# Moving the token-side sums of the down product and the last loads and stores before it in a fused attention and MoE kernel

## The reference

```
def _moe2_ref(x, w_in, w_out) -> np.ndarray:
    h = x @ w_in
    g = np.maximum(0.01 * h, h)
    return (g @ w_out).astype(np.float32)
```

## Time and profile before

| what | value |
|---|---|
| median of 3 runs | 822.38 us (821.12 to 822.7) |
| the profiled execution's own time | 823.07 us |
| its span in the trace | 821.2 us |
| PE busy | 805.5 us, 98% |
| DVE busy | 546.6 us, 67% |
| ACT busy | 457.7 us, 56% |
| POOL busy | 98.1 us, 12% |
| granted clock of PE over the span | 0.997 |
| DMA | 156.64 MB, mean 191 GB/s |

### The profile page before, as it was taken

How to read it: one execution, slowest core, us unless ns; L and a number is a source line. 1 busy time by engine, 2 the same in 40 slices (tenths; PEclk the granted TensorE clock), 3 DMA queues, 4 the chain that set the end, 5 groups by cost and what they waited for, 6 DMA issues and landing times.

```text
span 821.2 us, 13098 instructions
## 1 busy us (share of the span) xinstructions
PE 805.5 (98%) x4844; PEld 659.0 (80%) x4844; DVE 546.6 (67%) x906; ACT 457.7 (56%) x737; POOL 98.1 (12%) x220
## 2 busy tenths in 40 slices
PE   8889999999999999999999999999989999999998
PEld 6677778787888888888888888888868888888886
DVE  7778988877743285527643335665788699769775
ACT  4567777767743346345565446566744554555553
POOL 4454445432210000000000000000000000000000
PEclk9999999999999999999999999999999999999999
DMA  9675768665758876246684568445931840373002
GB/s 345 229 274 171 219 197 234 183 191 123 213 198 235 306 264 244 102 174 206 232 289 168 183 221 295 154 155 170 375 145 55 294 166 26 100 266 122 27 1 77
DMA packets 84496, 156.64 MB, mean 191 GB/s; under 512 B 6737, under 2 KB 35537, under 8 KB 84433
## 3 DMA queue, kind: packets, MB, share of 16 engines
q1 hardware_dynamic: 84432, 155.81, 56.6%
HBM read 99.16 MB, written 56.62 MB: 190 GB/s over the span
## 4 chain that ended last, share of the span: by engine, by line
PE 90%; DMA 3%; DVE 2%; issue 1%; POOL 1%; SPq 0%; ACT 0%; POOLq 0%; DVEq 0%
PE hid_a L731 22%; PE hid_b L731 21%; PE attn_ps L731 13%; PE scores_a L731 13%; PE scores_b L731 8%; PE probs_ps L731 7%; PE attn_ps L723 3%; DMA q_raw<-q_in 2%; DMA g_blk<-g_scratch 2%; PE probs_ps L709 2%; PE scores_a L697 1%; PE scores_b L697 1%; DVE ring_lo L1145 1%; DVE g_blk L1293 1%; POOL attn_buf L1435 0%
## 5 line engine op out<-in xcount | busy, mean ns | idle before, releaser
L862 ACT ACTIVATE ring_hi<-g_blk 128x512 fp32r<-128x512 f32 x168 | 105.9, 632 | 111.8 <-PE hid_a L731 42.5
L1145 DVE TENSOR_TENSOR ring_lo<-g_blk,ring_hi 128x512 fp32r<-128x512 f32 x168 | 115.2, 688 | 35.9 <-ACT ring_hi L862 32.6
L1009 ACT ACTIVATE g_out<-g_out 128x512 f32<-128x512 f32 x72 | 45.4, 630 | 71.4 <-DVE g_out L1272 41.1
L731 PE MATMUL hid_b<-ring_hi,w_hi 128*128 128x512 f32 x128 | 49.9, 390 | 0.2 <-DVE ring_lo L1145 0.2
L731 PE MATMUL hid_b<-ring_hi,w_lo 128*128 128x512 f32 x128 | 49.8, 389 | 0.0
L731 PE MATMUL hid_b<-ring_lo,w_hi 128*128 128x512 f32 x128 | 49.8, 389 | 0.0
L731 PE MATMUL hid_a<-w_in_hi,xT_hi 128*128 128x512 f32 x96 | 39.9, 416 | 4.0 <-DVE u L1191 3.3
L1145 DVE TENSOR_TENSOR w_lo<-w_raw,w_hi 128x1792 fp32r<-128x1792 f32 (+2 forms) x24 | 33.6, 1401 | 8.7 <-ACT w_hi L862 8.6
L731 PE MATMUL hid_b<-w_in_hi,xT_hi 128*128 128x512 f32 x96 | 39.3, 409 | 0.0
L1145 DVE TENSOR_TENSOR x_op_P_lo<-op_raw,x_op_P_hi 128x1024 fp32r<-128x1024 f32 x21 | 25.7, 1224 | 19.8 <-ACT x_op_P_hi L862 19.7
L901 ACT ACTIVATE u<-u,shift,gain 128x1024 f32<-128x1024 f32 x24 | 29.8, 1240 | 15.9 <-POOL shift L1455 15.8
(11 more groups left out here) (205 smaller groups left out, 2158.6 us busy)
## 6 DMA issues: line engine op xcount, KB each, us to landing
g_scratch<-g_out SPq DMA_DIRECT2D x96, 256.0 KB, 2.6
g_blk<-g_scratch SPq DMA_DIRECT2D x48, 512.0 KB, 7.2
attn_buf<-k_in SPq DMA_DIRECT2D x32, 384.0 KB, 5.6
attn_buf<-v_in SPq DMA_DIRECT2D x32, 384.0 KB, 3.9
ln_scratch<-lnT SPq DMA_DIRECT2D x24, 512.0 KB, 6.0
w_raw<-w_in SPq DMA_DIRECT2D x16, 512.0 KB, 4.2
q_raw<-q_in SPq DMA_DIRECT2D x32, 192.0 KB, 5.0
ln_even<-ln_scratch SPq DMA_DIRECT2D x12, 512.0 KB, 6.6
```

The costliest lines, as they stand in the source:

```text
L731: mm = pe.matmul(psum, weights[i], data[j], start=first and n == 0, stop=last and n == 2, skip_group_check=goes_on)
L862: return act.activation(dst, src, ACT.Copy)
L1009: act.activation(x, x, ACT.Prelu, alpha=0.01).then_inc(s_g[q], 1)
L1145: return ve.tensor_tensor(dst, x, hi.bitcast(f32), ALU.subtract)
```

## The change

It has two parts. No instruction is added or removed and no size changes.

**SP.** The store of the second last slice of block 12 (from `g_out0_12`) is issued behind four loads, not ahead of block 12's first load. The first two chunks of blocks 12 and 22 are loaded alternately. The last three stores (22, 21, 12 of the last slice) stand behind all loads, where before each stood between loads.

**DVE.** In span 0 the sums t3, t2 and t4 are formed later, and one (in P3's first slices one t3 and one t2) per step in place of two.

```diff
@@ sync engine, last iteration of up and behind it
                 if i == UPS - 1:
                     for c in range(4):
                         load_g(0, 21, c)
-                store_g(i - 1, 12)
+                    load_g(0, 12, 0)
+                else:
+                    store_g(i - 1, 12)
...
-            for c in (0, 1):
-                load_g(0, 12, c)
-            store_g(UPS - 1, 22)
-            for c in range(4):
+            load_g(0, 22, 0)
+            load_g(0, 12, 1)
+            load_g(0, 22, 1)
+            store_g(UPS - 2, 12)
+            for c in (2, 3):
                 load_g(0, 22, c)
-            store_g(UPS - 1, 21)
             for c in (2, 3):
                 load_g(0, 12, c)
-            store_g(UPS - 1, 12)
+            for q in (22, 21, 12):
+                store_g(UPS - 1, q)
@@ vector engine, behind ring_low of each down step
                 if b == 0:
-                    if p == "P2":
-                        t3(b, j)
+                    if p == "P2" and j >= 4:
+                        t3(b, j - 4)
                     elif p == "P3" and j < 4:
-                        t2(b, 2 * j)
-                        t2(b, 2 * j + 1)
+                        t3(b, j + 4)
+                        t2(b, j)
+                    elif p == "P6" and j < 4:
+                        t2(b, j + 4)
+                    elif p == "P6":
+                        t4(b, j - 4)
                     elif p == "P3":
-                        t4(b, 2 * j - 8)
-                        t4(b, 2 * j - 7)
+                        t4(b, j)
```

## The result

The changed kernel's median is 818.89 us (817.14 to 821.58, 22 runs); the kernel before had 821.95 (819.55 to 823.43, 22 runs) beside it. That is 3.1 us less by the medians. The ratio is 0.997, with a 95% interval of 0.9961 to 0.998: 2.5 us, 1.6 to 3.2 by the interval. I had forecast 2.8 us.

What follows compares the result with a forecast made beforehand. PE was taken as the bound, busy 805.5 of 821.2 us, so only its losses could be won: 4.16 us before less 1.35 after gives 2.8, median 822.4 to 819.6 us. Range 817.9 to 821.6.

Steps and rivals of the forecast that it cites:

- PE's loss in this place: From PE's first matmul of P2 (r = 8) to that of P7 (r = 32): 36.80 us, undisturbed 32.64, 4.16 lost.
- the stretch: Time on PE from the first matmul of P2 (r = 8) to that of P7 (r = 32), undisturbed 32.64 us.
- DVE's 30 operations: DVE's work from `ring_low` of r = 12 to that of r = 24: 30 at 0.602 us, 18.06 us.
- PE no longer waits at r = 9: 2.53 us come back.: PE's second step of P2: its late start, behind DVE's t3(0) waiting for a load, would go, returning 2.53 us.
- The chain of waits: Chain that ended last before: block 12's third load, landed at 603.43, then DVE's list up to P6.
- The store lands at L = 598.3: Store from `g_out0_12`, now behind four loads, lands at 598.3 us; ACT's second copy of P1's parts waits for it.
- the instruction packet: Instruction-queue packet at 595 to 596 us, holding one DMA engine 1.0 us; taken to delay the store from 597.3 to 598.3.
- 1.35: PE's remaining loss after the change, in us: 1.25 between r = 19 and r = 24, plus 0.1 for restarts.
- the rival without the packet: No wait to speak of at ACT: store lands at 597.3, gain 3.8 us (no wait 4.2), 818.6 to 818.2; chance 0.26.
- The slower rival: ACT waits for a store landing only with the queue's last, 605.4: 8.4 us lost, 826.7 us; chance 0.05.
- the break-even at 5.7 (L = 601.1): Gain was put at 601.1 less the store's landing time L, at most 4.2 us.
- the rule: PE's loss from r = 8 to r = 32 equals the start of ACT's second copy behind r = 8, less 1.64 us.

Runs made afterwards that it cites:

- t2 in pairs: Changed kernel with t3 still late, but t2 and t4 formed two per step as before: 820.34 us, ratio 0.9983 to the kernel before.

## Why the prediction was right, and where it was off

**PE's loss in this place is what there is to win.** Right: 4.16 us in the profile that I read, 3.44 in a second one. The gain in the stretch is 3.1 to 4.1 us between the profiles; the medians' 3.1 lies at its low end.

**DVE's order takes it away, and then DVE's 30 operations are the limit.** Right in mechanism and size: 18.07 us measured for 18.06, and the loss as a function of the copy's start fits at four points within 0.05 us. SP's order has no part in the gain that can be told: DVE's order alone reaches 0.9965, SP's alone 0.9991, and both together 0.9967.

**"PE no longer waits at r = 9: 2.53 us come back."** The split was wrong, though the sum was not. With SP's order alone the wait at r = 9 was gone, and 3.28 us were still lost. The old order is bound by t3(4) and by the sums behind it; the wait at r = 9 lies in the shadow of that, and is worth nothing while it stands. The chain of waits had said so: it ran through the load that landed at 603.43, and the prediction named it without pricing it. What counted was that t3(4) moved from ahead of `ring_low` of r = 13 to behind that of r = 16, and that t2 was spread.

**"The store lands at L = 598.3", with the instruction packet ahead of it.** This is the term that was mis-sized (2.9 us behind r = 8). The store landed 1.9 and 1.7 us behind r = 8, as the loads' pace alone gives. I had assumed two things: that the packet comes at a fixed place of PE's program, and that it adds about 1 us to a transfer behind it. Each failed in one profile. The queues' view for one us each shows the packet in the changed kernel from 592 to 593, some 2 us ahead of r = 8:

```profile
q1 hardware_dynamic: 120, 0.39, 98.5%
q8 instruction: 1, 0.02, 6.3%
```

So here it did come ahead of the store, and yet added nothing: the transfers around it landed (issue plus time to landing) at 590.6, 591.9, 593.2, 594.4 and 595.6, each about 1.25 us behind the one before, and the store at 596.3. In the second profile the packet is at 598 to 599, 1 to 2 us behind r = 8. The store landed at 598.5, and it was the load behind it that came late, at 600.7. With SP's order alone it is at 595 to 596, 0 to 1 us behind r = 8. There it did fall on the store: block 22's second load was issued at 584.9 and took 11.1 us, the store was issued at 585.3 and landed 2.1 us after that load, not 0.7:

```profile
L581 SPq DMA_DIRECT2D g_scratch<-g_out x1: 423/423/423, 585.3 to 585.3; - x1
...
DMA to landing us min/median/max: 12.8/12.8/12.8
```

So about the forecast delay can come, in some executions; in the two profiles of the changed kernel it did not. PE lost 0.30 and 0.08 us in place of 1.35, and since 0.08 is lost without any wait for the store too, ACT's wait cost about 0.2 us and nothing.

**Then why not 3.8 us?** That was the rival without the packet. Against the profile that I had read, the stretch did gain about that: 36.80 less 32.94 is 3.86. Against the second profile of before it is 3.1 to 3.4. In both profiles of the changed kernel PE also lost time at the first down step, 1 and 0.5 us, when ACT waited 2.3 and 1.8 us for block 11's first chunk. In the first profile:

```profile
578.85 1.15 ACT L865 ACTIVATE ring_hi<-g_blk 128x512 fp32r<-128x512 f32 x2 [2.35 <-DMA g_blk<-g_scratch]
```

With SP's order as in the changed kernel (t2 in pairs) that wait was 1.2 us and cost nothing, with the store last it did not occur, and in the other runs it was 0 to 1.4 and cost PE at most 0.1. SP's new order can't have made it either: in the changed kernel's two profiles the wait ended at 578.8 and 581.3, and the first transfer that stands elsewhere in the new order, block 12's first load, was issued only at 580.0 and 583.0. That it is chance is my reading, and how often it costs something in either kernel stays open. So the mechanism was right, but that the number came so close was partly luck. The forecast of 2.8 us had one large error, at least 1 us too much for the store. It was met by a loss before that can be 0.7 us smaller than I read, and by what PE lost at the first down step.

**The slower rival** was real as a mechanism, not as a case here: with the store behind all loads the time is above that of the kernel before, and with six loads ahead of it the gain is used up. There it landed about 5.0 us behind r = 8, where the prediction had put the break-even at 5.7 (L = 601.1); a loss before of 3.4 in place of 4.16 us accounts for the difference.

**Does a version beat both?** The changed kernel with the store first has 0.9963, DVE's order alone 0.9965, the changed one 0.9967 beside them. The three can't be told apart. In the two without ACT's wait for the store a late landing of it has nothing to spoil.

## What to carry to other kernels

- An engine that splits operands in list order delays its reader by the sum of all that stands between two of its steps. Count operations between two steps, times their pitch, and compare with the reader's pace. From the measured start of the first late operation this gave each loss here within 0.1 us. Foretold without that start it missed by over 1 us once (SP's order alone), because the landing under t3(4) was expected 1.5 us too early. Waits that the list of waits shows early may be worth nothing while a later one holds the same list.
- When a store is moved behind loads to get the loads sooner, look for who reuses its buffer. Here an early copy by ACT held the critical splits behind it, 1 us for 1 us once it started later than 1.6 us behind r = 8.
- Take the loss from two profiles before pricing a change of 0.3%: the same place lost 4.16 and 3.44 us.

## What had not been expected of the hardware

With the store last, PE stood still for 3.8 us. Its first matmuls behind it ran at the old speed, and then its granted clock fell to half, the 1.2 GHz level, for about 3.4 us. The columns are as above:

```profile
605.00:606.00 1.00, 0.69 (x3) 0.60 (x4) 1.00 (x3) 1.00 (x3) 0.00 (x0) 1.00 0.00 0
606.00:607.00 1.00, 1.00 (x5) 0.76 (x4) 1.00 (x3) 0.08 (x1) 0.00 (x0) 0.60 0.00 0
607.00:608.00 1.00, 1.00 (x4) 0.81 (x3) 1.00 (x3) 0.38 (x1) 0.00 (x0) 0.50 0.00 0
...
609.00:610.00 1.00, 1.00 (x5) 0.79 (x4) 1.00 (x3) 0.00 (x0) 0.00 (x0) 0.69 0.00 0
610.00:611.00 1.00, 1.00 (x6) 0.84 (x5) 1.00 (x3) 0.63 (x1) 0.00 (x0) 1.00 0.00 0
```

Behind the wait of 2.4 us in the kernel before it stayed at 1.00. The fall seems to have cost nothing in the end: 5.86 us were lost, and the rule, which knows only DVE's list up to r = 24, gives 5.88 without it.

An instruction packet of 0.02 MB took 6.3% of 16 DMA engines for 1 us, that is one engine for 1 us. In ten of the eleven profiles a landing at its place, or just behind it, came later than the pace of 1.25 us a load and 0.7 us a store gives: by 1.4 us with SP's order alone, by 0.8 to 1.3 us in five others, and by 0.2 to 0.7 us in the remaining four. In the changed kernel's first profile none did. That the packet is what holds the landing back is a reading of this coincidence; no run removed it. In both kernels its time differed by some 3 us between two executions, measured against PE's work.
